# Attention with an MLP beside it: two query tiles of all heads first, normalisation by two tiles, and the MLP from step 15 instead of 23

## What is computed

```python
k_all = concat([k_g, k_l]);  v_all = concat([v_g, v_l])
out_g = softmax(scale * q_g @ k_all.T) @ v_all            # 32 global queries
s_ll  = where(abs(i - j) <= 32, scale * q_l @ k_l.T, -1e9)  # 512 local queries
s_l   = concat([scale * q_l @ k_g.T, s_ll])
out_l = softmax(s_l) @ v_all
x   = concat([out_g, out_l]) -> (4, 544, 512), heads side by side
xn  = (x - mean) / sqrt(var + 1e-6) * g_ln
x   = x + relu(xn @ w_ch1) @ w_ch2                          # 512 -> 2048 -> 512
h   = relu(x @ w_in)                                        # 512 -> 1024
out = (h * sigmoid(conv3(h))) @ w_out
```

## Time and profile before

| what | value |
|---|---|
| median of three runs | 762.49 us (761.04 to 763.51) |
| the profiled execution: its time, its span | 762.49 us, 760.7 us |
| PE, weight loads, DVE, ACT, POOL busy | 746.1, 638.4, 336.3, 295.1, 139.3 us |
| mean granted TensorE clock | 0.995 of 2.4 GHz |
| DMA | 88.03 MB, 116 GB/s in the mean |
| first and last mixed step of MLP and attention | from 63.7 us to about 292 us |

### The profile page before, as it was taken

One profiled execution on the slowest core, in us unless ns is written; L12 is line 12 of the kernel. 1 busy time (PEld: TensorE's weight loads), 2 busy tenths in 40 slices (PEclk: granted clock), 3 DMA queues, 4 the chain that ended last, 5 costly groups with the idle time before them and its releaser, 6 DMA issues.

```text
span 760.7 us, 16627 instructions
## 1 busy us (share of the span) xinstructions
PE 746.1 (98%) x6802; PEld 638.4 (84%) x6802; DVE 336.3 (44%) x901; ACT 295.1 (39%) x758; POOL 139.3 (18%) x114
## 2 busy tenths in 40 slices
PE   8989999999999999999999999999989999999998
PEld 4656777777777778998989998888889999999997
DVE  4766434443354424422122222113167776677764
ACT  6977354453545442432122221111133433433343
POOL 0342000000000000432032430110202232223222
PEclk9999999999999999999999999999999999999999
DMA  9575414242253002362623683522533212221200
GB/s 329 177 275 167 149 49 161 60 121 92 65 177 112 4 29 98 113 193 73 205 68 107 187 262 114 168 82 63 160 116 114 74 46 89 62 88 34 86 31 30
DMA packets 84428, 88.03 MB, mean 116 GB/s; under 512 B 8832, under 2 KB 66432, under 8 KB 84352
## 3 DMA queue, kind: packets, MB, share of 16 engines
q1 hardware_dynamic: 83984, 86.37, 35.4%
q10 hardware_dynamic: 368, 0.59, 0.3%
HBM read 57.33 MB, written 29.62 MB: 114 GB/s over the span
## 4 chain that ended last, share of the span: by engine, by line
PE 94%; ACT 2%; DVE 1%; DMA 1%; issue 1%; POOL 0%; ACTq 0%; DVEq 0%
PE u_ps L513 38%; PE y_ps L513 27%; PE s_ps L513 17%; PE t_ps L554 6%; PE o_ps L513 5%; DMA identf<-in_ident 1%; PE u_ps L554 1%; ACT e_sb L926 1%; ACT probs L952 0%; ACT w_hi L986 0%; ACT e_sb L929 0%; POOL hb L1093 0%; ACT xn L968 0%; ACT y_sb L1033 0%; DVE xn L752 0%
## 5 line engine op out<-in xcount | busy, mean ns | idle before, releaser
L841 DVE SCALAR_TENSOR_TENSOR hb<-u_ps,hb 128x384 fp32r<-128x384 f32 (+1 forms) x48 | 28.9, 602 | 175.9 <-ACT hb L996 175.9
L513 PE MATMUL u_ps<-xc,w_hi 128*128 128x274 f32 x512 | 100.2, 290 | 0.0
L996 ACT ACTIVATE hb<-u_ps 128x384 fp32r<-128x384 f32 (+1 forms) x48 | 25.3, 527 | 175.4 <-PE u_ps L513 175.4
L858 DVE SCALAR_TENSOR_TENSOR conv_h<-relu_h,conv_sb,conv_h 128x272 f32<-128x272 f32 x128 | 88.7, 693 | 4.6
L513 PE MATMUL u_ps<-xn,w_hi 128*128 128x256 f32 x448 | 86.6, 291 | 0.1
L1093 POOL TENSOR_TENSOR hb<-gated,hb 128x272 fp32r<-128x272 f32 x64 | 54.9, 858 | 156.4 <-ACT hb L1026 156.4
L513 PEld LDWEIGHTS u_ps<-xc,w_hi 128*128 128x128 f32 x512 | 81.5, 190 | 0.2
L952 ACT COPY probs<-t_ps 128x512 f32<-128x512 f32 (+1 forms) x67 | 36.5, 546 | 103.5 <-PE t_ps L554 103.3
L1078 POOL TENSOR_TENSOR w_lo<-w_raw,w_hi 128x1024 fp32r<-128x1024 f32 x22 | 52.6, 2390 | 127.9 <-ACT w_hi L986 127.9
L513 PE MATMUL u_ps<-xc,w_lo 128*128 128x274 f32 x256 | 74.5, 291 | 0.0
L1012 ACT ACTIVATE relu_h<-u_ps 128x274 f32<-128x274 f32 x64 | 25.7, 401 | 122.0 <-PE u_ps L513 122.0
(11 more groups left out here) (109 smaller groups left out, 1505.8 us busy)
## 6 DMA issues: line engine op xcount, KB each, us to landing
w_raw<-in_wall SPq DMA_DIRECT2D x22, 512.0 KB, 3.8
two<-in_kq SPq DMA_DIRECT2D x15, 640.0 KB, 5.9
xc<-y_parts SPq DMA_DIRECT2D x8, 1092.0 KB, 5.8
vv<-in_vx SPq DMA_DIRECT2D x16, 520.0 KB, 6.5
y_parts<-yT SPq DMA_DIRECT2D x16, 512.0 KB, 3.5
xn_parts<-xn SPq DMA_DIRECT2D x14, 512.0 KB, 3.4
xb<-xn_parts SPq DMA_DIRECT2D x14, 512.0 KB, 6.6
y_first<-y_sb SPq DMA_DIRECT2D x17, 256.0 KB, 4.8
```

What stands on the lines that cost most here:

```text
L513: return nc.tensor.matmul(out, lhsT, rhs, start=start, stop=stop)
L841: v.scalar_tensor_tensor(out=lo, in0=u_ps[n % 2][:, 0:width], scalar=0.0, in1=hi.bitcast(f32), op0=ALU.max, op1=ALU.subtract).then_inc(hlo ...
L858: v.scalar_tensor_tensor(out=cv, in0=h[:, n:CN + n], scalar=conv_sb[:, f, n:n + 1], in1=cv, op0=ALU.mult, op1=ALU.add).then_inc(cv_ok, 1)
L996: nc.scalar.activation(h_parts(n)[0], u_ps[n % 2][:, 0:width], ACT.Relu).then_inc(hhi_ok, 1)
```

## The change

Six things move together, all by tables and small functions:

- `place(s)`: unit s is now, within a batch, the tiles 0 and 1 of all four pairs of heads, then the tiles 2 and 3 of all four. So the first two tiles of a batch are complete after eight units instead of thirteen or more.
- `SLOTS` goes from 4 to 8 and `PSLOTS` from 4 to 5; loads of `two` and `vv` are issued nine or ten steps ahead of `first_use`.
- The norm works by two tiles (`stats_before`, `half_sums(c, half)`, `variances(c)`, `inverse_deviation(c)`), with semaphores and a column of its own for the global tile; `ln_step(t)` is 8(t//2)+13+t%2 and GT is on step 68.
- `U0` is 15 instead of 23, so the first MLP begins eight steps earlier and the loop is eight steps shorter.
- Burst, G0, G1 and values of group G stand on steps 8G+2, +4, +5 and +7.
- `W_STEP`, the weights' steps, follow. In ACT the exponentials now stand ahead of the group's. PE's order inside a step stays.

```diff
-SLOTS, PSLOTS, HSLOTS = 4, 4, 3
-U0 = 23
+SLOTS, PSLOTS, HSLOTS = 8, 5, 3
+U0 = 15
...
+def place(s):
+    b, r = divmod(s, 16)
+    u, r = divmod(r, 8)
+    return 4 * b + r // 2, 2 * u + r % 2
+GT_STEP = 68
 def ln_step(t):
-    return 75 if t == GT else 16 * (t // QT + 1) + 5 + t % QT
+    return GT_STEP if t == GT else 8 * (t // 2) + 13 + t % 2
...
-    if s % 8 == 1 and 0 <= (s - 9) // 8 < NGROUPS:
-        found.append(("G0", (s - 9) // 8))
-    if s % 8 == 2 and 0 <= (s - 10) // 8 < NGROUPS:
-        found.append(("G1", (s - 10) // 8))
+    if s % 8 == 4 and s // 8 < NGROUPS:
+        found.append(("G0", s // 8))
+    if s % 8 == 5 and s // 8 < NGROUPS:
+        found.append(("G1", s // 8))
...
 def burst_in(s):
-    return s // 8 - 1 if s % 8 == 0 and 0 <= s // 8 - 1 < NGROUPS else None
+    return s // 8 if s % 8 == 2 and s // 8 < NGROUPS else None
...
-W_STEP = ([5, 7, 9, 13, 15, 17, 21, 23] + [70 + 2 * j for j in range(8)]
+W_STEP = ([7, 9, 11, 13, 15, 16, 17, 19] + [67 + 2 * j for j in range(8)]
...
             def load_two(p):
                 if p >= SLOTS:
-                    sp.wait_ge(gs_ok, (p - SLOTS) // 2 + 1)
+                    sp.wait_ge(s_ok, last_use(p - SLOTS) + 1)
...
             def load_xg():
-                sp.wait_ge(pv_ok, len(V_SEQ))
...
+            load_two(2)
             load_v(1)
+            load_two(3)
+            load_v(2)
...
-                for p in range(2, TWOS):
-                    if 4 * p - 8 == s:
+                for p in range(4, TWOS):
+                    if first_use(p) - 10 == s:
                         load_two(p)
...
-                p, t = divmod(s, QT)
+                p, t = place(s)
...
-            def inverse_deviation(b):
-                n = 1 if b == BATCH else QT
-                pool.wait_ge(stat_ok, stats_before(b) + (3 if b == BATCH else 13))
+            def inverse_deviation(c):
+                at = 2 * (c % 2)
+                pool.wait_ge(stat_ok, stats_before(c + 1))
+                if c >= 2:
+                    pool.wait_ge(lnn_ok, 2 * (c - 1))
```

More of the change, by code:

```diff
@@ L78, in global_values_in @@
 def global_values_in(s):
-    return (s - 11) // 8 if s % 8 == 3 and 0 <= (s - 11) // 8 < NGROUPS else None
+    return s // 8 if s % 8 == 7 and s // 8 < NGROUPS else None
 def burst_in(s):
-    return s // 8 - 1 if s % 8 == 0 and 0 <= s // 8 - 1 < NGROUPS else None
+    return s // 8 if s % 8 == 2 and s // 8 < NGROUPS else None
 T_SEQ, T_STEP = [], []
@@ L102, in score_bank @@
 def score_bank(s):
-    return int(s < U0 and s % 2 == 1 and s not in (9, 17))
+    return int(s < U0 and s % 2 == 1 and s not in (3, 11))
 def score_before(s):
@@ L129, in o_head @@
 def o_head(m):
-    return m + m // GH
+    return m + (m + 2) // GH
 def o_group(G):
-    return 5 * G + 4
-O_FLIP = 10
+    return 5 * G + 2
+O_FLIP = 6
 def o_bank(k):
@@ L471, in _ @@
             for s in range(END):
-                for p in range(2, TWOS):
-                    if 4 * p - 8 == s:
+                for p in range(4, TWOS):
+                    if first_use(p) - 10 == s:
                         load_two(p)
-                    if v_load_step(p) == s:
+                for p in range(3, TWOS):
+                    if max(first_use(p) - 9, 0) == s:
                         load_v(p)
+                for e in range(TILES):
+                    c = min(e // 2, 7)
+                    if s == U0 + HALF * (c + 1) + 2:
+                        store_y1(e)
                 for j in range(24):
@@ L489, in _ @@
                         store_xn(t)
[L490 to L493, removed]
                 for k in range(1, len(CH2)):
-                    if s == (0, 77, 90, 104, 112)[k]:
+                    if s == U0 + (0, 54, 67, 81, 89)[k]:
                         load_xb(k)
@@ L520, in scores @@
                     pe.wait_ge(bias_ok, 2 * (score_before(s) + 1))
[L521 to L524, removed]
+                if burst_in(s) is not None and burst_in(s) >= 2:
+                    pe.wait_ge(gexp_ok, burst_in(s) + 1)
+                if s in (5, 13):
+                    pe.wait_ge(gexp_ok, s // 8 + 1)
                 for j in range(2):
@@ L576, in values @@
             def values(gp):
-                p, t = divmod(gp, QT)
+                p, t = place(gp)
                 k = o_head(gp // 2)
@@ L803, in variances, with half_sums @@
-            def variances(b):
-                n, halves = (1, 1) if b == BATCH else (QT, 2)
-                dve.wait_ge(stat_ok, stats_before(b) + n * halves)
+            def half_sums(c, half):
+                dve.wait_ge(o_ok, o_head(4 * c + 2 * half + 1) + 1)
+                for t in (2 * c, 2 * c + 1):
+                    v.bn_stats(bst[:, t % QT, half, :],
+                               x_loc[c // 2 % 2][:, t % QT, 256 * half:256 * (half + 1)]).then_inc(stat_ok, 1)
+            def variances(c):
+                at = 2 * (c % 2)
+                dve.wait_ge(stat_ok, stats_before(c) + 4)
+                v.memset(bn_gate[:, :], 0.0)
+                for t in (at, at + 1):
+                    v.bn_aggr(mv[:, t, :], bst[:, t, 0:2, :].rearrange("p a b -> p (a b)")).then_inc(stat_ok, 1)
+                dve.wait_ge(stat_ok, stats_before(c) + 6)
+                v.tensor_scalar_add(veps[:, at:at + 2], mv[:, at:at + 2, 1], 1e-6).then_inc(stat_ok, 1)
@@ L806, in variances, with global_variances @@
+            def global_variances():
+                dve.wait_ge(xg_in, 16)
+                v.bn_stats(bst[:, QT, 0, :], x_g[:, :]).then_inc(gstat_ok, 1)
+                dve.wait_ge(gstat_ok, 1)
                 v.memset(bn_gate[:, :], 0.0)
[L807 to L810, removed]
+                v.bn_aggr(mv[:, QT, :], bst[:, QT, 0, :]).then_inc(gstat_ok, 1)
+                dve.wait_ge(gstat_ok, 2)
+                v.tensor_scalar_add(veps[:, QT:QT + 1], mv[:, QT:QT + 1, 1], 1e-6).then_inc(gstat_ok, 1)
@@ L812, in ln_rows @@
             def ln_rows(t):
-                b, r = divmod(t, QT)
+                b, r = (0, QT) if t == GT else divmod(t, QT)
                 i = LN_ORDER.index(t)
-                dve.wait_ge(rstd_ok, b + 1)
+                if t == GT:
+                    dve.wait_ge(grstd_ok, 1)
+                else:
+                    dve.wait_ge(rstd_ok, t // 2 + 1)
                 if i >= 2:
@@ L880, in _ @@
                 for t in range(TILES):
-                    if s == ln_step(t) - 1 - (t == GT) - (t % QT == 1):
+                    if s == ln_step(t) - 1 - (t != GT and t % 2):
                         ln_rows(t)
@@ L900, in _ @@
                     read_out((s - 4) // 2)
[L901 to L908, removed]
+                if s % 8 == 7 and s // 8 < 2 * BATCH:
+                    half_sums(s // 8, 0)
+                if s % 8 == 3 and 1 <= s // 8 <= 2 * BATCH:
+                    half_sums(s // 8 - 1, 1)
+                    variances(s // 8 - 1)
+                if s == GT_STEP - 2:
+                    global_variances()
                 if s in W_AT and W_AT[s] < 2 * HALF:
@@ L1047, in _ @@
                     probabilities(("T", s - 2))
+                if s < PAIRS and not late:
+                    exponents(s)
                 if G is not None:
                     global_exponents(G)
-                if s < PAIRS and not late:
-                    exponents(s)
                 if 0 <= s - U0 < N1 + N2:
@@ L1098, in _ @@
                     weights_lo(W_AT[s - 1])
[L1099 to L1102, removed]
+                if s % 8 == 3 and 1 <= s // 8 <= 2 * BATCH:
+                    inverse_deviation(s // 8 - 1)
+                if s == GT_STEP - 2:
+                    global_inverse_deviation()
                 if 0 <= s - 2 - C0 < CUNITS:
```

56 lines of the change are left out of this document (29 added, 27 removed).

## The result

| | before | after |
|---|---|---|
| median | 761.8 us | 769.3 us (four runs, 768.48 to 769.56) |
| profiled span | 760.7 us | 767.4 us |
| ratio after/before | | 1.0093, 95% interval 1.0073 to 1.0114 |

The change is slower by 0.9%, as forecast (768.8; range 763.5 to 772.0). The medians of before in this document come from runs on the same chip as the kernel beside them, so they differ a little (761.8 to 762.6). The two spans differ by 6.7 us, the sum of the terms was 6.3. The medians differ by 7.5, as the profiled execution of before (762.49) lies above its median.

What follows compares the result with a forecast made beforehand. TensorE was taken as the bound, with room only in the first 63.7 us (lead-in). Terms 1.8 + 5.0 - 0.9 + 0.4 = +6.3 took the span from 760.7 to 767.0, time 768.8 us, range 763.5 to 772.

Steps and rivals of the forecast that it cites:

- term 2: Beside the MLP, the norm's transpose waits for the group transpose G1's copy in one bank: 0.83 us, six times, +5.0 us.
- terms 3: Lead-in before the MLP: first up at 48.3 us against 49.2 for 63.7 less eight steps, -0.9 us.
- 4: Small items: the last norm tile, one MLP-only step before its up, is late by +0.4 us; the others nothing.
- Term 1: Eight attention steps move from the lead-in (1.81 us each) to beside the MLP (4.85 against 2.82): +1.8 us.
- the walk: Lead-in traced wait by wait: PE loses 6.7 us over a floor of 40.1, first up at 46.8 before the clock's part.
- the low clock: One low-clock stretch in the lead-in, added to the walk: 1.5 us, between 0 and 3.1.
- A: Rival: the new waits at the norm's transposes are hidden, 763.8 us, no change; chance 0.11.
- B: Rival: lead-in waits go, PE runs at its floor, first up at 40.6: 761.1 or 758.6 us; chance 0.06.
- C: Rival: lead-in steps are half-filled by weight loads, so moved ones give back 46%, 6.7 us: 762.1 us; chance 0.05.
- D: Rival: a second low-clock stretch into the first MLP steps, or DVE held by a late weight: 772.3 us; chance 0.15.

Runs made afterwards that it cites:

- experiment 6: Changed kernel, group transposes one step earlier and values ahead of the transposes: 754.95 us; kernel before with only values ahead: 757.75 us.
- experiment 1: Changed kernel with both group transposes one step earlier from the third group on, never in a step with the norm's transpose: 762.49 us.
- experiment 2: Changed kernel with both group transposes one step later from the third group on, each ahead of a norm transpose: 774.65 us.
- experiment 5: Changed kernel with the keys of pair 1 loaded ahead of the values of pair 0: 768.16 us.
- experiment 4: Changed kernel with weight casts moved out of the second group's steps (weights' steps 7, 8, 14 to 19): 766.39 us.
- experiment 7: Changed kernel with groups apart, values ahead, moved weight casts and earlier key load: 753.35 us; with the eighth cast at step 20: 753.55 us.

## Why the prediction was right, and where not

The sign, the mechanism and the total (6.3 foreseen, 6.7 measured) hold. That the total is so close is partly luck: term 2 was 1.2 too small, terms 3 and 4 together 0.7 too high, and the executions of before on record lie between 759.7 and 764.5 us. Term by term:

- **Term 1 (+1.8): right.** Mixed steps stayed at 4.84 and 4.85. The rule of the Trainium skill (TensorE: Matmul & The Clock Gate, "Back-to-back issue gap"), by which alternating has no price, did not describe this kernel's order; the step of 4.63 in experiment 6 agrees with it in its sum, but there, too, blocks cost more or less by their neighbours, and the differences cancel.
- **Term 2 (+5.0): mechanism right, size too small.** Six waits, at the places named and of 0.82 to 0.83 each, but each meeting costs 1.03, so the term is 6.2. The step that failed is "LN starts at 123.26 instead of 122.43: 0.83 us": it counted how much later LN starts and took the rest of the step as unchanged, but LN is 0.89 late by the starts, and two transposes that meet save the early start behind up once instead of twice (experiments 1 and 2).
- **Term 3 (-0.9): total nearly right by luck, two parts off against each other.** The first up came at 47.96, 1.24 before 49.2, where 48.3 was said. The waits of the walk were 1.05, 0.5, 1.05, 1.15, 0.9 and 1.85, with the key load's 0.45 a sum of 6.95, though the walk says 6.7. The timeline lists 0.75, 0.49, 0.77, 1.19, none and 1.48. The key load cost 9.90 - 9.10 = 0.8, not 0.45, as it landed 7.6 us after its issue. These listed losses are 5.5, but the first up lies 7.9 behind the walk's floor of 40.1. With the clock's part below taken off, 7.3 to 7.5 remain where the walk had 6.7: by the starts the waits cost more than the list says, as in experiment 1. And **"that is 1.5 us"** for the low clock was too much. The clock did fall, at the forecast place:

```profile
39.00:44.00 5.00, 4.48 (x60) 3.19 (x64) 2.99 (x11) 2.79 (x9) 2.34 (x1) 0.66 0.93 333
```

The kernel of experiment 2 is the same up to step 15, and in its profile the clock stayed at 1.00 over these 5 us. There the waits are longer instead (its PE):

```profile
42.65 0.63 PE L573 MATMUL t_ps<-identf,ln_n 128*128 128x128 f32 x4 [0.57 <-DVE xn L771]
...
46.16 0.63 PE L573 MATMUL t_ps<-identf,e_sb 128*128 128x128 f32 x4 [1.61 <-DVE xn L771]
...
47.52 0.51 PE L530 MATMUL u_ps<-xn,w_hi 128*128 128x256 f32 x2
```

From the start of step 2 to the first up it takes 37.51 us there (from 10.01) and 38.06 after (from 9.90). Two more kernels have the same code there: from LN's start to the first up it takes 7.88 us in experiments 2 and 5, with the clock at 1.00, 8.44 after, and 8.21 in the first kernel of experiment 1, which has 0.66 too. The clock level itself cost 0.3 to 0.6 us: PE works slower in time that it would otherwise wait, because the chain over ACT, DVE and POOL sets the end. My sum added a cost of PE to a walk in which PE was not the bound.
- **Term 4 (+0.4): not there.** The timelines of PE and DVE at the last norm tile:

```profile
333.66 0.48 PE L529 MATMUL y_ps<-w_hi,h_hi 128*128 128x512 f32 x1
...
335.36 0.61 PE L529 MATMUL u_ps<-xl,w_hi 128*128 128x384 f32 x2
```

```profile
334.62 0.69 DVE L770 TENSOR_TENSOR xl<-t_ps,xl 128x512 fp32r<-128x512 f32 x1 [0.27 <-ACT xl L992]
```

The up waits for the subtraction that ends at 335.31, and starts 0.22 late (1.70 behind the down's start instead of 1.48). But the kernel before had the same 0.22 once, at the place of the earlier trace rows (down at 302.84, up at 304.54). I had read the duration there without asking whether a step already waited for it.
- Sum with the measured sizes: 1.8 + 6.2 - 1.2 + 0 = 6.8, against 6.7 between the spans.
- **Rivals.** A (waits hidden) fell with the six rows. B (lead-in at its floor, 40.6) fell with the first up at 47.96, though experiments 4, 5 and 7 went 3.8 of the 7.4 us towards it. C gave 762.1 by steps that do not grow; they grew, but experiment 6 shows that they need not. Its reason, that the share of weight loads leaves room in the lead-in's steps, found no support: in the order of experiment 6 the moved steps take 1.81, as in the lead-in, and not 46% less. D's held-up DVE did occur (a multiply of 2.83 us at 54.88 after) and did not reach PE, which had slack there.

## What to carry over

Where a table puts work on steps, check for each pair of items in one step whether they use one buffer, and what the engine that empties it has ahead of that in its order; price the meeting by the length of the whole step, not by the listed wait. In a stream where two kinds of matmul alternate, time each block from start to start by who stands behind whom: here one permutation inside the step (4.5 to 7.5 us) was worth more than moving eight steps. Where another engine's chain sets the end, do not add the cost of a slower clock to it in full.

## What was not expected of the hardware

- **A TensorE block costs by its neighbour.** Up starts 0.41 us behind the four transposes, values 0.58. Up took 0.10 more with values behind it than with down (1.61 against 1.51), down 0.12 more with values ahead of it than with up (1.60 against 1.48), and none of it stood in a wait list.
- **DVE's multiply of two SBUF tensors and POOL's subtraction exclude each other.** After:

```profile
54.88 2.83 DVE L851 TENSOR_TENSOR y_sb<-y_sb,g_sb 128x512 f32<-128x512 f32 x1
```

```profile
54.78 2.38 POOL L1102 TENSOR_TENSOR w_lo<-w_raw,w_hi 128x1024 fp32r<-128x1024 f32 x1 [5.64 <-ACT w_hi L1010]
```

POOL ends at 57.16 and the multiply, 0.68 us long, at 57.71. In the trace of before the first eight multiplies meet no subtraction and take 0.68 or 0.69; three later ones start in the last 0.2 to 0.5 us of one (at 316.37, 322.45 and 328.09), take 0.77, 1.04 and 0.77, and each ends 0.55 behind it. The other way round, in experiment 7 a multiply that starts at 47.28 takes 0.67, and the subtraction that starts at 47.26 takes 2.96 instead of 2.38. The Trainium skill (SBUF — State Buffer, "SBUF: two separate sides") says that a VectorE operation with two SBUF inputs and a GpSimd operation share a port pair that one of them holds for its whole instruction; the rows agree, at 2.83 and 2.88 us.
- **A low clock cost 0.3 to 0.6 us and not 1.5** over five microseconds at 0.66, as told under term 3.
